# Windowed attention and two MLPs on one core: tiles of 384 tokens become one of 256 and four of 512, with attention steps of four blocks

## What is computed

```python
B, H, S, D = 4, 8, 576, 64                    # attention, window of 64
scores = q @ k.T / sqrt(D)                    # per batch and head
scores = where((i - j >= 0) & (i - j < 64), scores, -1e9)
attn = exp(scores - max);  attn /= attn.sum() + 1e-9
x = (attn @ v) laid out as [B * S, H * D]     # 2304 tokens of 512
h = maximum(maximum(x @ w1, x @ w2), x @ w3)  # 512 -> 768
x = h @ w_out                                 # 768 -> 512
h = x @ w_in                                  # 512 -> 2048
g = where(h >= 1, h, where(h <= -1, 0, (h + 1)**2 / 4))
y = g @ moe2_w_out                            # 2048 -> 512
```

## Time and profile before

| | |
|---|---|
| time, three runs | 860.85, 860.96 (median), 861.62 us |
| span of the profiled execution | 858.9 us (its own time isn't listed apart; the median is 2.1 above the span) |
| TensorE busy | 812.4 us, 95% of the span |
| TensorE weight load busy | 760.4 us, 89% |
| VectorE, ScalarE, GpSimd busy | 390.7, 367.1, 300.4 us (45%, 43%, 35%) |
| DMA | 39.65 MB, 46 GB/s over the span |
| granted TensorE clock | 9 or more tenths in every slice of the page |

### The profile page before, as it was taken

One profiled execution on the slowest core, in us unless ns is written; L12 is line 12 of the kernel. 1 busy time (PEld: TensorE's weight loads), 2 busy tenths in 40 slices (PEclk: granted clock), 3 DMA queues, 4 the chain that ended last, 5 costly groups with the idle time before them and its releaser, 6 DMA issues.

```text
span 858.9 us, 13859 instructions
## 1 busy us (share of the span) xinstructions
PE 812.4 (95%) x4464; PEld 760.4 (89%) x4464; DVE 390.7 (45%) x1003; ACT 367.1 (43%) x881; POOL 300.4 (35%) x266
## 2 busy tenths in 40 slices
PE   4769998999999989999999999999999999999998
PEld 3669998988898989999999999999999999999997
DVE  6878868768778687131222222222222222222221
ACT  6666565465464553215534323323323233333222
POOL 3644334234243332606604522322332332332221
PEclk9999999999999999999999999999999999999999
DMA  6611212111212121204310000000000000000000
GB/s 223 221 41 40 78 39 77 56 58 41 73 38 76 38 87 42 74 2 138 115 39 25 1 1 37 0 0 37 0 0 37 0 0 37 0 0 37 0 0 37
DMA packets 17942, 39.65 MB, mean 46 GB/s; under 512 B 1920, under 2 KB 8064, under 8 KB 17920
## 3 DMA queue, kind: packets, MB, share of 16 engines
q1 hardware_dynamic: 17920, 39.39, 13.9%
HBM read 34.67 MB, written 4.72 MB: 46 GB/s over the span
## 4 chain that ended last, share of the span: by engine, by line
PE 75%; DVE 12%; issue 5%; ACT 4%; DMA 2%; DVEq 1%; SPq 0%; ACTq 0%; POOL 0%
PE bank L421 23%; PE wide L432 23%; PE bank L379 15%; PE bank L407 9%; PE wide L354 2%; DVE qT L587 2%; DVE masked L605 2%; ACT prob L475 2%; DMA k_in<-k_dram 2%; DVE x_rest L587 1%; DVE masked L613 1%; DVE pT L587 1%; DVE xT L633 1%; DVE row_inv L619 1%; DVE h L643 1%
## 5 line engine op out<-in xcount | busy, mean ns | idle before, releaser
L379 PE MATMUL bank<-xT,w 128*128 (+1 forms) x1296 | 249.4, 344 | 2.7 <-DVE xT L633 2.7
L379 PEld LDWEIGHTS bank<-xT,w 128*128 128x128 f32 x1296 | 225.5, 191 | 4.3 <-issue 3.4
L421 PE MATMUL bank<-yT,w 128*128 x1152 | 215.3, 337 | 0.0
L432 PE MATMUL wide<-w,gT 128*128 128x512 f32 x864 | 212.9, 393 | 0.0
L421 PEld LDWEIGHTS bank<-yT,w 128*128 128x128 f32 x1152 | 204.2, 188 | 7.3
L693 POOL TENSOR_TENSOR gT<-g,gT 128x384 fp32r<-128x384 f32 x96 | 97.6, 1017 | 296.0 <-ACT gT L451 296.0
L432 PEld LDWEIGHTS wide<-w,gT 128*128 128x128 f32 x864 | 161.0, 188 | 29.7
L685 DVE TENSOR_SCALAR g_sq<-bank 128x384 f32<-128x384 f32 x96 | 53.5, 557 | 228.1 <-PE bank L421 227.8
L554 ACT ACTIVATE g_sq<-g_sq,half 128x384 f32<-128x384 f32 x96 | 59.2, 616 | 189.2 <-DVE g_sq L685 188.8
L688 DVE TENSOR_TENSOR g<-bank,g_sq 128x384 f32<-128x384 f32 x96 | 53.5, 558 | 71.3 <-ACT g_sq L554 59.0
L693 POOL TENSOR_TENSOR v_part<-v_nat,v_part 128x384 fp32r<-128x384 f32 x48 | 49.5, 1030 | 104.2 <-ACT v_part L451 104.2
(11 more groups left out here) (46 smaller groups left out, 751.5 us busy)
## 6 DMA issues: line engine op xcount, KB each, us to landing
v_nat<-v_dram SPq DMA_DIRECT2D x24, 384.0 KB, 3.1
stage<-w_dram SPq DMA_DIRECT2D x16, 512.0 KB, 3.4
k_in<-k_dram SPq DMA_DIRECT2D x24, 224.0 KB, 3.2
q_in<-q_dram SPq DMA_DIRECT2D x24, 192.0 KB, 3.2
h<-moe_w_dram SPq DMA_DIRECT2D x12, 384.0 KB, 6.0
out_dram<-o_sb SPq DMA_DIRECT2D x18, 256.0 KB, 2.1
stage<-moe_w_out_dram SPq DMA_DIRECT2D x1, 1536.0 KB, 7.6
mask<-masks_dram SPq DMA_DIRECT2D x1, 320.0 KB, 5.6
```

The costliest lines, as they stand in the source:

```text
L379: mm = pe.matmul(acc[gr % 2][:, 0:TOK], w123[:, wp, w, kc, c * P:(c + 1) * P], xT[:, of(t, 0), xp, kc, :].rearrange("p a n -> p (a n)"), s ...
L421: mm = pe.matmul(acc3[f % 4][:, 0:TOK], w34[:, f, wp, kc * P:(kc + 1) * P], yT[:, of(t, 1), yp, kc, :].rearrange("p a n -> p (a n)"), star ...
L432: mm = pe.matmul(acc4[tb], gT[:, f % 4, gp, tb * P:(tb + 1) * P], w34[:, f, wp, DM:2 * DM], start=(f == x == 0), stop=(f == C2 - 1 and x = ...
```

## The change

Attention and layer 1 have their own tiling: one first tile of FIRST_TOK = 256 tokens, then four of BIG_TOK = 512 (BIGS = 5 tiles in all, where TILES was 6). A step has SB = 4 blocks (256 tokens), so that the first tile has four steps, one for each pair, and each of the others eight, as before two for a pair: 36 steps instead of 48. Layer 1 matmuls have 256 columns in the first tile and 512 in the others; they are 1080 instead of 1296. Layers 2 to 4 keep tiles of 384 (MTOK).

The tile `masked` is gone: the mask is added into `prob`, and the exponential is taken in place. VectorE's add therefore waits for the transposes of two steps ago (`p_turned`) where it waited for their exponentials, and ScalarE's wait for `p_turned` goes. The masks are 2 x SB blocks (0.5 MB), and a step chooses its part by `mask_place`.

The places of the steps are new; values of the last step now stand ahead of the last group of the stage instead of behind it. The first stage is written out by itself, since its layer 1 tile is the small one. Five pieces of w1 to w3 are split ahead of it (before: eight) and seven in its slots (before: four), the latter all by VectorE.

v is loaded by steps, each load waiting until the step two back has split its own. SP issues the second weight matrix after the loads of pairs 2 and 3 and the third after the first loads of the next tile. xT is larger (512 tokens, two buffers), and the layer 2 weights and their staging place now lie where attention's buffers were: their load waits for the last xT of all, and GpSimd's copy of them also for layer 1 of all tiles but the last.

```diff
-TOK = 384
-SB = 3
-PARTS = NB // SB
+MTOK = 384
+TOK = 256
+SB = NB
+STEP_TOK = TOK
+PARTS = 2
+BIG_TOK = PARTS * TOK
+FIRST_TOK = TOK
+BIGS = 1 + (N - FIRST_TOK) // BIG_TOK
-SCORE_AT = (2, 3, 5, 7, 9, 10, 12, 14)
-AFTER = {"score": 0, "norm": 1, "v": 2, "probs": 3, "values": 4}
-QK_AT, QK_AT_FIRST = (0, 1, 3, 8), (0, 1, 3, 5)
+SCORE_AT = (1, 3, 5, 7, 9, 11, 13, 14)
+AFTER = {"score": 0, "norm": 1, "v": 1, "probs": 2, "values": 3}
+QK_AT = (0, 2, 6, 10)
...
+FIRST = [[] for _ in range(PAIRS + 1 + max(AFTER_FIRST.values()))]
+for _u in range(PAIRS):
+    FIRST[_u].append(("qk", _u))
+    for _kind in AFTER_FIRST:
+        FIRST[1 + _u + AFTER_FIRST[_kind]].append((_kind, _u))
...
-HI_FIRST = {2: (0,), 5: (1,), 7: (2,), 9: (3,), 10: (4, 5, 6, 7)}
-HI_SLOT = {4: (8,), 6: (9,), 9: (10, 11)}
-POOL_FIRST, POOL_SLOT = {4: (0,), 6: (1,), 7: (2,), 10: (5,)}, {}
-DVE_FIRST, DVE_SLOT = {9: (3,), 10: (4, 6, 7)}, {5: (8,), 6: (9,), 10: (10, 11)}
+HI_FIRST = {2: (0,), 3: (1,), 4: (2,), 5: (3,), 6: (4,)}
+HI_SLOT = {0: (5,), 1: (6,), 2: (7,), 4: (8,), 6: (9,), 8: (10,), 10: (11,)}
+POOL_FIRST, POOL_SLOT = {4: (0,), 5: (1,)}, {}
+DVE_FIRST, DVE_SLOT = {5: (2, 3), 6: (4,)}, {1: (5,), 2: (6,), 3: (7,), 5: (8,), 7: (9,), 9: (10,), 11: (11,)}
...
+    for part in range(cols // STEP_TOK):
+        i = part + u * (cols // STEP_TOK)
+        after(sp, v_lo, step_of(a, i) - 1)
+        sp.dma_start(v_nat[:, i % 2, :, :].rearrange("p j n -> p (j n)"),
+                     v[ds(piece_of(a, part) * PAIRS + u, 1), :, :].rearrange("a p n -> (a p) n"))\
+            .then_inc(v_landed[i], 16)
...
-        for n in range(3):
-            weights(n)
-            if n + 2 < PAIRS:
-                loads(0, n + 2)
+        weights(0)
+        loads(0, 2)
+        loads(0, 3)
+        weights(1)
+        loads(1, 0)
+        weights(2)
+        for u in range(1, PAIRS):
+            loads(1, u)
...
+        sp.wait_ge(x_lo, 2 * ALL_STEPS)
         sp.dma_start(stage[:, 0:C1 * DM].rearrange("p (c n) -> p c n", c=C1),
...
-                    after(act, p_turned, s - PARTS + 1)
-                        act.activation(prob[:, part, b, :], masked[:, part, b, :], ACT.Exp,
+                        act.activation(prob[:, i % 2, b, :], prob[:, i % 2, b, :], ACT.Exp,
...
-                    after(dve, exped, SB * (s - PARTS + 1))
+                    after(dve, p_turned, s - 1)
...
-                    dve.tensor_tensor(masked[:, part, :, :], s_ps[:, :, 1, :],
+                    dve.tensor_tensor(prob[:, i % 2, :, :], s_ps[:, :, 1, :],
...
-        pool.wait_ge(x_lo, 2 * STEPS * TILES)
+        pool.wait_ge(x_lo, 2 * ALL_STEPS)
+        pool.wait_ge(l1_done, GROUPS * (BIGS - 1))
```

More of the change, by code:

```diff
@@ L149, in attention_mlp_kernel @@
     x_rest, at = place("x_rest", [P, STEP_TOK], F32, at)
-    mask, at = place("mask", [P, (SB + PERIOD - 1) * SPAN], F32, at)
+    mask, at = place("mask", [P, 2 * SB * SPAN], F32, at)
     ident, at = place("ident", [P, P], F32, at)
-    neg_max, at = place("neg_max", [P, PARTS, 4], F32, at)
-    row_sum, at = place("row_sum", [P, PARTS, 4], F32, at)
-    row_inv, A_END = place("row_inv", [P, PARTS, 4], F32, at)
+    neg_max, at = place("neg_max", [P, PARTS, SB], F32, at)
+    row_sum, at = place("row_sum", [P, PARTS, SB], F32, at)
+    row_inv, A_END = place("row_inv", [P, PARTS, SB], F32, at)
+    A_AT = X_AT + 4 * 2 * 2 * KC * MTOK
     wo1, at = place("wo1", [P, 2, C1, DM], F32R, A_AT)
[L158 to L162, removed]
+    h1s, H1S_END = place("h1s", [P, 2, 2, C1, MTOK], F32R, at)
+    stage, at = place("stage", [P, 3 * 2 * DM], F32, H1S_END)
+    half, at = place("half", [P, 8], F32, max(at, A_END))
+    assert at <= nc.sbuf_usable_end and A_END <= nc.sbuf_usable_end
     w34, at = place("w34", [P, C2, 2, 2 * DM], F32R, W_AT)
     EARLY = (A_AT - W_AT) // (2 * 2 * DM * 4)
[L166 to L172, removed]
+    g_sq, at = place("g_sq", [P, MTOK], F32, at)
+    g, at = place("g", [P, MTOK], F32, at)
+    yT, at = place("yT", [P, 2, 2, KC, MTOK], F32R, H1S_END - 4 * 2 * 2 * KC * MTOK)
+    assert g is not None and H1S_END - 4 * 2 * 2 * KC * MTOK >= W_AT + 4 * C2 * 4 * DM + 2 * 4 * MTOK
+    gT, at = place("gT", [P, 4, 2, MTOK], F32R, H_AT + KC * N * 4)
     o_sb, at = place("o_sb", [P, QB, DM], F32, at)
@@ L387, in _ @@
             attention(0, plan)
-        with pe.Fori(0, TILES - 1) as t:
+        for slot in range(SLOTS):
+            attention(1, PLAN[slot])
+            layer1(0, slot)
+        attention(1, PLAN[SLOTS])
+        with pe.Fori(1, BIGS - 1) as t:
             for slot in range(SLOTS):
@@ L406, in _ @@
                     for x, (wp, hp) in enumerate(PASSES):
-                        mm = pe.matmul(acc[c % 2][:, 0:TOK], wo1[:, wp, kc, c * P:(c + 1) * P],
+                        mm = pe.matmul(acc[c % 2][:, 0:MTOK], wo1[:, wp, kc, c * P:(c + 1) * P],
                                        h1s[:, of(t, 1), hp, kc, :].rearrange("p a n -> p (a n)"),
@@ L438, in _ @@
         LAG = 2
-        with pe.Fori(0, TILES) as t:
+        with pe.Fori(0, MTILES) as t:
             for f in range(C2):
@@ L501, in _ @@
                 weights_hi(*divmod(piece, KC))
-        for first, last in ((0, 1), (1, TILES - 1)):
-            with act.Fori(first, last) as t:
-                for slot in range(SLOTS):
-                    attention(t + 1, PLAN[slot])
-                    if slot < C1:
-                        layer1(t, slot)
-                    for piece in HI_SLOT.get(slot, ()) if first == 0 else ():
-                        weights_hi(*divmod(piece, KC))
-                attention(t + 1, PLAN[SLOTS])
-        with act.Fori(TILES - 1, TILES) as t:
+        for slot in range(SLOTS):
+            attention(1, PLAN[slot])
+            if slot < C1:
+                layer1(0, slot)
+            for piece in HI_SLOT.get(slot, ()):
+                weights_hi(*divmod(piece, KC))
+        attention(1, PLAN[SLOTS])
+        with act.Fori(1, BIGS - 1) as t:
+            for slot in range(SLOTS):
+                attention(t + 1, PLAN[slot])
+                if slot < C1:
+                    layer1(t, slot)
+            attention(t + 1, PLAN[SLOTS])
+        with act.Fori(BIGS - 1, BIGS) as t:
             for gr in range(C1):
@@ L566, in rows_out @@
                 act.activation(o_sb[:, tb, :], acc4[tb], ACT.Copy).then_inc(o_out, 1)
-        for first, last in ((0, 1), (1, TILES - 1)):
+        for first, last in ((0, 1), (1, MTILES - 1)):
             with act.Fori(first, last) as t:
@@ L725, in _ @@
                 weights_lo(*divmod(piece, KC))
-        for first, last in ((0, 1), (1, TILES - 1)):
-            with pool.Fori(first, last) as t:
-                for slot in range(SLOTS + 1):
-                    attention(t + 1, PLAN[slot])
-                    for piece in POOL_SLOT.get(slot, ()) if first == 0 else ():
-                        weights_lo(*divmod(piece, KC))
-        pool.wait_ge(x_lo, 2 * STEPS * TILES)
+        for slot in range(SLOTS + 1):
+            attention(1, PLAN[slot])
+            for piece in POOL_SLOT.get(slot, ()):
+                weights_lo(*divmod(piece, KC))
+        with pool.Fori(1, BIGS - 1) as t:
+            for slot in range(SLOTS + 1):
+                attention(t + 1, PLAN[slot])
+        pool.wait_ge(x_lo, 2 * ALL_STEPS)
+        pool.wait_ge(l1_done, GROUPS * (BIGS - 1))
         pool.wait_ge(wo1_in, 16)
```

289 lines of the change are left out of this document (159 added, 130 removed).

## The result

The changed kernel takes 887.38 us (median of 4 runs, 886.24 to 888.35), before 860.9: a ratio of 1.0308 (1.0291 to 1.0324). Forecast were 851 us and, at the outside, 862. The profiled execution took 886.24, its span is 884.3.

What follows compares the result with a forecast made beforehand. Full stages were taken as bound by TensorE's columns, the first stage by VectorE. First stage's end at 106, plus 3 x 71.3, plus last stage 49.9, gave 369.8 against 379.6, 9.8 us less: 851 us, range 843 to 862.

Steps and rivals of the forecast that it cites:

- a matmul costs its columns: TensorE's full streams: time goes by columns, about 0.45 ns each, so widening a full stream saves under 1%.
- the prologue: Before the first stage: VectorE gets through it at 44.5 us instead of 58.2, 13.7 saved.
- priced at nothing, in place: Attention's exponential in place: VectorE's add waits for transposes already done at least one slot ahead; cost nothing.
- the three signs of being wrong: Late k loads on SP inside stages, 512-wide qT splits over 1.5 us each, or a first stage over 70 us.
- the walk of the full stages: Three 512-token stages: following the plan slot by slot gives 3.2 us of waits each, so 71.3 us a stage.
- the rival: Clock falls in the first stage: 17 us more if wholly slow (78.9 instead of 62), time 868; chance 0.08.
- the sum of TensorE's work: Each full stage: layer 1 matmuls 51.2 and attention 16.9, together 68.1 us.
- VectorE is the bound, and TensorE's work hides beneath it: First stage: VectorE's 59.6 us of work plus 2.4 of waits make 62, above TensorE's 43.0.
- waits that grow with the columns: Rival for the stages: waits get 4/3 longer, 4.3 us slower or near no change, 860 to 865; chance 0.13.
- The rule cited there: Skill's rule on TensorE's clock: bursts after long enough idle gaps restart low, putting the first stage toward 79 us.
- its even spacing: Steps spread evenly over slots, argument for a rival with stages near TensorE's own pace (69), 840 to 846; chance 0.15.

Runs made afterwards that it cites:

- e4: The kernel before with only the exponential in place added, the mask being added into prob; 858.43 us, ratio 0.9976.
- e13: The changed kernel with the qk of pairs 1, 2 and 3 at slots 3, 7 and 11 instead of 2, 6 and 10; 862.38 us.
- e9: e6 with the low parts of the first stage's seven weight pieces made by GpSimd instead of VectorE; 861.87 us.
- e6: The changed kernel with transposes three and values four slots behind scores, scores at the old slots, first two qk at slots 0 and 1; 862.42 us.
- e2: The changed kernel with extra useless 512-column matmuls ahead of the values of steps 0, 2 and 4; 872.77 us.
- e18: The changed kernel with e6's slots in the first stage and e13's in the full stages; 859.69 us, ratio 0.9992.
- e1: The changed kernel with VectorE splitting pT ahead of the mask add and maximum instead of behind them; 869.47 us.
- e14: e13 with VectorE's pT split ahead of the mask add, as in e1; 892.21 us, ratio 1.0360.
- e3: The kernel before (384 tokens, three blocks) with the changed kernel's slots alone; 887.89 us, ratio 1.0312.
- e11: e9 and e10 together, on e6's plan; 864.38 us, ratio 1.0046.
- e10: e6 with ten extra useless 512-column matmuls at each of three idle places of TensorE in the first stage; 861.39 us.

## Why the prediction was wrong

What bounds the kernel was read rightly: a matmul costs its columns (the last stage 49.3 for 216 of 512 columns, forecast 49.9), the tail is unchanged, and the prologue came out 2.2 us from its sum. The last part of the change I priced at nothing, in place, was a gain where it could be tried alone (e4). Two of the three signs of being wrong came: the first stage took over 70 us, and qT splits took 1.49 to 1.68 us each, where 1.5 was the limit.

The step that failed is the walk of the full stages: "TensorE wants it at 11.85. One us late, twice." The mechanism and two of its places, slots 8 and 12, were right; three terms were short. From the start of slot 5 at 217.29 the qT split ended at 11.0 and not 9.9: beside GpSimd's kT and v it took 3.20, where the walk had 2.65 and the prediction 3.1 as the worst, and x ended 0.3 later. With h, add, maxima and the whole pT the values could start at 14.3, asked for at 12.0. So the two places cost 2.31 and 2.35. Second, slot 4 (1.47 us) and slot 17 (0.57) were taken as free; at slot 2 VectorE itself waited 1.85 for ScalarE's half of qT, which the walk had not followed. Together 6.7 us instead of 3.2. Third, the slow pitch behind the two waits of over 2 us, 3.3 a stage, which the rival had put into the first stage alone. 68.1 + 6.7 + 3.3 is 78.1, measured 78.6. e13 shows that the sum of TensorE's work was nearly sound: a stage of 71.8 with waits of 2.7 leaves 69.1, forecast 68.1.

In the first stage the step "VectorE is the bound, and TensorE's work hides beneath it" failed. Its sum was 59.6, and it was busy for 54.4 of the 73.2, so the sizes were not too small: the two engines took turns. Behind pT come values, a group and scores on TensorE, and VectorE's next add waits for them (1.91 us at 68.45), as TensorE waited 4.7 before that. e9 fits it, on e6's plan: less work for VectorE, no shorter stage. By TensorE's own account the stage is 20.7 us of idle time and 52.6 busy, where the forecast had 19 and 43.0. So TensorE's idle time was nearly as forecast, and its work was not: it ran at the low level for 21.9 of the 73.2 us, 7.5 of them at the stage's start. Some of that may only stand in the place of waiting for VectorE. What ending some of it gave back is 5.7 (e2), a third of the 17 that the rival had for a wholly slow stage. How the 11.7 us over the forecast divide between turns and clock stays open beyond that.

The rivals: waits that grow with the columns did not happen (e13, e18). The clock was real, but small by itself. In the full stages e1 and e13 end it by ending the long waits; in the first stage the mean granted clock stayed at 0.83 (e1) and 0.86 (e13). The rule cited there from the Trainium skill, "TensorE: Matmul & The Clock Gate", section on HAM oscillation, is that bursts with long enough idle gaps start at the low clock again. It agrees with the trace in that slow matmuls stand behind waits (2.31, 2.35 and 4.41 us here). But the length of the wait alone doesn't decide it. Behind another wait of 2.31 us, in the second stage at 154.43, twelve matmuls took the usual 2.81, while the clock fell behind 1.71 us in the kernel before and behind 1.21 in e14 (at 223.26). What decided, that the plan of slots is worse at the old width too (e3), was not among the rivals; I had read its even spacing as a help.

Why the gain of the widths is so small even when cured (e18): the prologue is 9.7 shorter, but the first stage is 10.1 longer; it has attention for 512 tokens beside layer 1 for 256, where before had 384 beside 384. The rest up to layer 2, with the 128 tokens of layer 1 that the first stage left over, takes 263.1 us, against 264.9 before.

Open: why the first stage takes 68 in e6 and 74 in e13, whose full stages are the shorter ones, and why e11 is over 4 us worse there than e9 and e10; why the clock fell behind some waits and not behind others as long. Not tried: GpSimd's splits moved away from qT with the order left alone, and the exponential not in place at the new widths.

## What to carry to other kernels

In a plan written by hand, place the long piece of a helper engine behind the product that the main engine asks for next, and check it in every slot with the helper's measured worst time; one slot's shift was worth 25 us of 887 here, and the tile widths gave nothing that could be told from the kernel before (e18). A sum of busy time bounds a stage only if no engine waits for the other's answer within a step: follow one round trip first. An idle stretch on TensorE has to be priced with the slow matmuls behind it.

## What was not expected of the hardware

The granted clock fell inside a stage in which TensorE was 91% busy (71.83 of 78.70 us), behind a single wait of 2.31 us at 172.5. TensorE had had no other wait since 154.43. A wait of 0.98 us behind the extra matmuls did not do it (e2), and one of 2.91 had not in the kernel before, yet one of 1.71 had.

Extra matmuls of no use, 18 for each full stage and 48 for the first, made the kernel 15 us faster.

A qT split of 64 x 512 took VectorE 0.67 to 0.69 us while GpSimd was idle and 1.49 to 1.68 while GpSimd made its own splits, so that the two of a pair took 1.39 us at 46.73, 2.22 in e13's slots and 3.20 at the place of the change.
